# An attention and mixing kernel: GpSimd rotates q and k ahead of splitting v, and the orders of four engines change

## The chip, the cores and the metric

One NeuronCore of one Trainium2 chip runs the whole kernel. The metric is the time of one execution in microseconds (us), measured on the device; less is better. The core has five engines that run their own instruction streams and meet through semaphores: TensorE (PE; its weight loads are shown as PEld), VectorE (DVE), ScalarE (ACT), GpSimd (POOL) and SyncE (SP), which here only issues DMA transfers.

## What is computed

```python
# q, k, v: (4, 8, 576, 64) float32; H * D = 512
q_rot, k_rot = rotate(q), rotate(k)            # rotary positions: halves times cos and sin
scores = (1 / sqrt(D)) * q_rot @ k_rot^T
attn = exp(scores - max(scores))
attn = attn / (sum(attn) + 1e-9)
x = (attn @ v)  as (4, 576, 512)
xk, xr = mu * x + (1 - mu) * x_prev            # mu_k and mu_r; x_prev is x shifted by one row
x = sigmoid(xr @ w_r) * (relu(xk @ w_k)**2 @ w_v)
u = x + token mixing of x (w_tok1, relu, w_tok2)
out = u + relu(u @ w_ch1) @ w_ch2
```

All inputs and the output are float32. Products are made in three matmuls of rounded high parts and low rests, so most operands are split into a "hi" (rounded, by ScalarE or GpSimd) and a "lo" (the rest, by VectorE or GpSimd).

## The kernel before, in words

The 32 heads go through a software pipeline of slots. In slot h, the kernel scores head h, weighs head h - 1 (turns its probabilities and multiplies them with v), and prepares head h + 1 (transposes its rotated q and k and splits them). GpSimd rotates q and k still earlier. Two slots, `slot(it, 0)` and `slot(it, 1)`, make one turn of the loops over `it`; slots 0, 1, 30, 31 and the last one, which only weighs, are written outside of the loop. Behind the 32 heads come the gated part, the token mixing and the channel mixing, which the change doesn't touch.

The order of an engine's work in a slot is written by hand as a string, lines 65 to 67. A letter is a kind of work and a digit is which tile or unit of it:
- For TensorE (`ORDER`): T turns a unit of the last head's probabilities (8 units, line 606), S scores one of five tiles of queries (line 588), P prepares the next head: P0 transposes q and the last keys (lines 572, 573) and P1 the other keys (line 577), V weighs a unit (lines 620 and 626). V0 reads v unsplit (`raw_v`), V1 to V7 the split `v_pair`. All V wait for the split of v, by a wait in front of V0.
- For ScalarE (`ACT_ORDER`): H rounds a turned unit (line 850), P0 to P3 round the transposed keys and q (lines 816, 820, 824), E is the exponential of a tile with its sum (line 837), O copies the low part of an output span (line 855), v rounds v of this slot's head (line 861, into `v_pair`).
- For VectorE (`DVE_ORDER`): I adds 1e-9 to the last head's sums and inverts them (lines 1078, 1080), M is the maximum of a tile (line 1054), L the rest of a turned unit (line 1071), P0 to P3 the rests of q and k (lines 1027, 1033, 1038), O adds an output span into `xT` (line 1088).

Two score tiles and two turned units have PSUM banks at a time, so S2 waits for E0, S3 for E1, T2 for H0, T3 for L1, and so on.

GpSimd's order is the function `slots` (lines 514 to 523). `split_v` (line 490) makes the low part of v and waits for ScalarE's v. `rotate` (lines 481 to 486) makes the rotated q and k of the head two ahead; it waits for the load of that head and for the transposes (P1) of the head that used the same buffer. TensorE's P0 waits for it. `split_w1_hi` and `split_w1_lo` (lines 498, 501) split a piece of the gated part's weights; the first waits until n loads of weights have landed. `scale_x` (line 507) multiplies two finished heads in `xT` by the inverse sums that were read back.

SyncE issues all transfers of the loop in one order, `slots` of its block: for each head `sums_out` (line 376: the inverse sums, 5 x 128 numbers of 4 bytes, into DRAM; waits for the inversion), `next_v` (lines 366 and 368: v of the head two on; waits until the weighing of V0 and the split have freed the buffer), `sums_back` (line 384: reads the sums back, repeated over 64 partitions; waits for their landing in DRAM and, for even heads, for `scale_x` of the pair before), on one side of the pair a load of weights (line 372, the first ten pairs), and `next_qk` (lines 362, 363: q and k of the head four or five on; waits for the rotation that frees the buffer). A wait holds everything behind it in the queue:

```python
def sums_back(it, kk, first=False):
    sp.wait_ge(sums_stored, it * 32 + (16 * kk + 16))
    if i == 0 and not first:
        sp.wait_ge(x_scaled, it)
    sp.dma_start(rb[...], sum_rows[...]).then_inc(rb_in, 16)
```

Of the kernel before, what the change touches and what calls it, by code (L numbers as in the profile page):

```python
# [14 lines left out]
def attention_rwkv_mixer(nc: bass.Bass, q, k, v, mu_k, mu_r, w_k, w_v, w_r,  # L15
# [43 lines left out]
    def steps(text):  # L59
        return [(x[0], int(x[1])) for x in text.split()]  # L60
# [1 line left out]

    ORDER = steps("T0 T1 S0 P0 S1 T2 V0 T3 V1 S2 T4 V2 T5 S3 P1 T6 V3 T7 S4 V5 V4 V6 V7")
    ACT_ORDER = steps("H0 H1 P0 P1 P2 H2 E0 H3 E1 H4 O0 H5 E2 v0 H6 H7 P3 E3 O1 E4")
    DVE_ORDER = steps("I0 M0 L0 L1 M1 P0 L2 P1 L3 M2 P2 L4 O0 L5 M3 L6 L7 M4 P3 O1")

    LAST_ORDER = steps("T0 T1 V0 V1 T2 T3 V2 T4 V3 K0 T5 V4 K1 T6 V5 K2 T7 V6 K3 V7")
    LAST_ACT_ORDER = steps("H0 H1 X0 H2 X1 H3 O0 X2 H4 X3 H5 X4 H6 X5 H7 X6 O1 X7")  # L70
# [6 lines left out]
    with ExitStack() as ctx:  # L77
# [223 lines left out]
        def upto(it, kk, n, c):  # L301

            return it * (2 * n) + (n * kk + c)
# [21 lines left out]
        def rope_half(rot, by_cos, by_sin, j, h):  # L325

            half = D // 2
            a = by_cos[:, j, :, h * half:(h + 1) * half]
            b = by_sin[:, j, :, (1 - h) * half:(2 - h) * half]
            if j == 0:  # L330
                return rot[:, 0:NT, h * half:(h + 1) * half], a, b
            return (rot[:, :, :, h * half:(h + 1) * half], a.unsqueeze(2).to_broadcast([P, NT, 2, half]),
                    b.unsqueeze(2).to_broadcast([P, NT, 2, half]))

        def both(table):
            return table[:, :, :].unsqueeze(1).to_broadcast([P, 2, NT, D])
# [131 lines left out]
        @block.gpsimd  # L468
        def _(pool):
            g = nc.gpsimd  # L470
            pool.wait_ge(zeros_ready, 1)
            g.affine_select(out=ident[:, :], in_=ident[:, :], compare_op=ALU.not_equal, fill=1.0, base=0,
                            pattern=[[-1, P]], channel_multiplier=1).then_inc(ident_ready, 1)

            def rotate(it, i, kk, first):

                pool.wait_ge(qk_in[i], it * 64 + (64 * (kk // 2) + 64))
                if not first:
                    pool.wait_ge(prep_turned, upto(it, kk - 2, 2, 2))
                    pool.wait_ge(k_roped, upto(it, kk, 1, 0))  # L480
                g.tensor_tensor(times_cos[:, :, :, :], raw_qk[i][:, :, :, :], both(cos), ALU.mult).then_inc(rope_step, 1)  # L481
                g.tensor_tensor(times_sin[:, :, :, :], raw_qk[i][:, :, :, :], both(sin), ALU.mult).then_inc(rope_step, 1)  # L482
                pool.wait_ge(rope_step, upto(it, kk - 1, 2, 2))
                for j, (rot, done) in enumerate(((rot_q[i], q_roped), (rot_k[i], k_roped))):
                    g.tensor_tensor(*rope_half(rot, times_cos, times_sin, j, 0), ALU.subtract)
                    g.tensor_tensor(*rope_half(rot, times_cos, times_sin, j, 1), ALU.add).then_inc(done, 1)  # L486

            def split_v(it, i, kk):
                pool.wait_ge(v_hi_ready, upto(it, kk, 1, 1))
                g.tensor_tensor(v_pair[i][:, :, D:P], raw_v[i][:, :, 0:D], v_pair[i][:, :, 0:D], ALU.subtract).then_inc(v_lo_ready, 1)  # L490

            def piece(it):
                return bass.ds(it * PIECE, PIECE)

            def split_w1_hi(it, n):

                pool.wait_ge(w1_in, n * 16)
                g.tensor_copy(w1_hi[:, piece(it)], w1_raw[:, piece(it)]).then_inc(w_hi, 1)

            def split_w1_lo(it):  # L500
                g.tensor_tensor(w1_lo[:, piece(it)], w1_raw[:, piece(it)], w1_hi[:, piece(it)], ALU.subtract).then_inc(w_lo, 1)  # L501

            def scale_x(p):
                pool.wait_ge(span_out, p * 4 + 4)
                pool.wait_ge(rb_in, p * 32 + 32)
                at = bass.ds(p * COLS + 1, S)
                g.tensor_tensor(xT[:, at], xT[:, at], rb[:, :], ALU.mult).then_inc(x_scaled, 1)

            pool.sem_inc(q_roped, 1)
            pool.sem_inc(k_roped, 1)  # L510
            pool.wait_ge(tables_in, 32)
            rotate(0, 1, 1, True)

            def slots(it, n, scaling):
                split_v(it, 0, 0)
                rotate(it, 0, 2, False)
                split_w1_hi(it, n)
                pool.wait_ge(w_hi, it + 1)
                split_v(it, 1, 1)
                split_w1_lo(it)  # L520
                rotate(it, 1, 3, False)
                if scaling:
                    scale_x(it - 1)

            slots(0, 1, False)
            with pool.Fori(1, N_WV) as it:
                slots(it, it + 1, True)
            with pool.Fori(N_WV, HEADS // 2 - 1) as it:
                slots(it, N_WV, True)
            last = HEADS // 2 - 1  # L530
            split_v(last, 0, 0)
            for n in range(last, HALF_UNITS):
                split_w1_hi(n, N_WV)
                pool.wait_ge(w_hi, n + 1)
                split_w1_lo(n)
                if n == last:
                    split_v(last, 1, 1)
                if n == last + 2:
                    scale_x(last - 1)
            scale_x(last)  # L540


            for n, (size, sources, hi, lo, _) in enumerate(TOK_UNITS):
                pool.wait_ge(tok_w_in[n], 16 * len(sources))
                g.tensor_copy(hi, stage_w[:, n, 0:size]).then_inc(w_hi, 1)
                pool.wait_ge(w_hi, HALF_UNITS + n + 1)
                g.tensor_tensor(lo, stage_w[:, n, 0:size], hi, ALU.subtract).then_inc(w_lo, 1)


            with pool.Fori(0, B) as b:  # L550
                for j, (hi, lo) in enumerate(((wc1_hi, wc1_lo), (wc2_hi, wc2_lo))):
                    at = bass.ds(b * STAGE, STAGE)
                    pool.wait_ge(ch_w_hi, b * 2 + (j + 1))
                    g.tensor_tensor(lo[:, at], stage_w[:, j, :], hi[:, at], ALU.subtract).then_inc(w_lo, 1)  # L554
# [3 lines left out]
        def _(pe):  # L558
# [95 lines left out]

            def slot(it, kk, scoring=True, weighing=True, preparing=True, order=ORDER):

                i = kk % 2
                first_score = isinstance(it, int) and it == 0 and kk == 0
                for what, n in order:
                    if what == "S" and scoring:  # L660
                        score(it, i, kk, n, first_score)
                    elif what == "T" and weighing:
                        turn(it, 1 - i, kk - 1, n, weighing == "first")
                    elif what == "V" and weighing:
                        weigh(it, 1 - i, kk - 1, n, weighing == "first")
                    elif what == "K":
                        if n == 0:
                            pe.wait_ge(w_lo, KD * FF // PIECE)
                        gated_k(0, n)
                    elif what == "P" and preparing:  # L670
                        prepare(it, 1 - i, kk + 1, n)
# [139 lines left out]
        def _(act):  # L811
# [69 lines left out]

            def slot(it, kk, scoring=True, weighing=True, preparing=True, first=False, order=ACT_ORDER):
                i = kk % 2
                for what, n in order:
                    if what == "X":
                        if n == 0:
                            wait_for_room(act)
                            act.wait_ge(omu_ready, 1)
                            act.wait_ge(x_scaled, KD)
                        mix2(0, 0, n, after=False)  # L890
                    if what == "E" and scoring:
                        exponent(it, i, kk, n)
                    elif what == "H" and weighing:
                        hi_part(it, kk - 1, n)
                    elif what == "O" and weighing:
                        copy_o_lo(it, 1 - i, kk - 1, n)
                    elif what == "v" and scoring:
                        values_hi(it, i, kk, first)
                    elif what == "P" and preparing:
                        prep(it, 1 - i, kk + 1, n)  # L900
# [120 lines left out]
        def _(dve):  # L1021
# [86 lines left out]

            def slot(it, kk, scoring=True, weighing=True, preparing=True, first=False, order=DVE_ORDER):
                i = kk % 2  # L1110
# [190 lines left out]
```

## Time and profile before

| | us |
|---|---|
| median of 3 runs | 1166.11 (1163.17 to 1166.35) |
| the profiled execution, its own time | 1165.27 |
| its span, first to last instruction | 1163.1 |
| busy: TensorE | 1016.8 |
| busy: VectorE | 636.4 |
| busy: ScalarE | 537.0 |
| busy: GpSimd | 298.0 |

The span is counted from the first to the last instruction of the profiled execution; its time holds 2.17 us more. "Busy" leaves out waits. The granted clock (PEclk) is the share of 2.4 GHz that TensorE was given, so 0.50 is 1.2 GHz. In the timeline a bracket behind a row gives the idle time of the engine before it and what ended it.

### The profile page before, as it was taken

The numbers are of one execution on the slowest core, as the hardware profiler recorded it, in microseconds if no ns is written. First come the engines' busy times: TensorE is split into PE (matmuls) and PEld (weight loads), VectorE is DVE, ScalarE is ACT, GpSimd is POOL, SyncE is SP. The second block draws the span as 40 slices with busy tenths as digits, with TensorE's granted clock in tenths as the row PEclk, the third lists the DMA queues.
The fourth block names the chain that finished last, engine by engine and source line by source line (L and its number), as shares of the span: only waits on it lengthen the run. The fifth ranks groups of instructions, "written<-read, shape, count | busy, mean of one in ns | idle before, by whom it ended". The sixth has DMA issues, their size and how long they took to land.

```text
span 1163.1 us, 21141 instructions
## 1 busy us (share of the span) xinstructions
PE 1016.8 (87%) x6976; PEld 961.7 (83%) x6976; DVE 636.4 (55%) x1232; ACT 537.0 (46%) x1280; POOL 298.0 (26%) x291
## 2 busy tenths in 40 slices
PE   4877777777777777879999999999999999999998
PEld 3766666666776666779999999988899999999997
DVE  5666666667666666779777777744522122212211
ACT  3666666666666666764444434435312112211210
POOL 4454555554544455442000000024200000000000
PEclk9888888998888888889999999999999999999999
DMA  3122222222222121111000000003000000000000
GB/s 81 38 60 58 60 57 52 53 60 60 60 42 42 40 39 31 22 47 62 1 0 0 0 0 0 0 28 108 28 1 21 21 1 20 20 20 0 20 20 20
DMA packets 93629, 37.70 MB, mean 32 GB/s; under 512 B 84000, under 2 KB 84896, under 8 KB 93600
## 3 DMA queue, kind: packets, MB, share of 16 engines
q1 hardware_dynamic: 93312, 37.00, 12.9%
q10 hardware_dynamic: 288, 0.33, 0.1%
q8 instruction: 16, 0.26, 0.1%
q14 instruction: 13, 0.11, 0.1%
HBM read 32.51 MB, written 4.80 MB: 32 GB/s over the span
## 4 chain that ended last, share of the span: by engine, by line
PE 66%; issue 14%; POOL 11%; ACT 5%; DVE 3%; POOLq 0%; DMA 0%; ACTq 0%; SPq 0%; DVEq 0%
PE psum L635 17%; PE psum L637 17%; PE psum L636 17%; PE psum L588 4%; POOL times_cos L481 3%; POOL times_sin L482 3%; PE psum L620 3%; PE psum L606 3%; POOL w_lo L501 2%; PE psum L572 2%; PE psum L626 2%; ACT probs L837 1%; ACT pT_hi L850 1%; POOL rot_q L486 1%; PE psum L723 1%
## 5 line engine op out<-in xcount | busy, mean ns | idle before, releaser
L1054 DVE TENSOR_REDUCE neg_max<-psum 128x1 f32<-128x576 f32 (+1 forms) x160 | 120.5, 753 | 120.8 <-PE psum L588 112.0
L1003 ACT ACTIVATE h_hi<-psum 128x288 fp32r<-128x288 f32 x96 | 39.5, 411 | 245.8 <-PE psum L637 245.8
L606 PE MATMUL psum<-ident,probs 128*128 128x128 f32 x800 | 137.9, 295 | 2.4 <-issue 2.3
L572 PE MATMUL psum<-ident,rot_q 128*128 128x128 f32 x96 | 24.7, 387 | 117.6 <-issue 109.1
L850 ACT ACTIVATE pT_hi<-psum 128x320 fp32r<-128x320 f32 (+3 forms) x224 | 100.7, 450 | 42.7 <-PE psum L606 38.9
L837 ACT ACTIVATE probs<-psum,neg_max 128x576 f32<-128x576 f32 (+1 forms) x160 | 118.0, 737 | 3.6 <-DVE neg_max L1054 2.0
L606 PEld LDWEIGHTS psum<-ident,probs 128*128 128x128 f32 x800 | 103.3, 151 | 17.9 <-issue 8.6
L588 PE MATMUL psum<-kT_hi,qT 128*128 128x288 f32 x320 | 111.3, 360 | 7.4 <-DVE kT_lo L1038 5.6
L572 PEld LDWEIGHTS psum<-ident,rot_q 128*128 128x128 f32 x96 | 14.4, 192 | 123.7 <-issue 123.7
L635 PE MATMUL psum<-u_hi,wc_hi 128*128 128x288 f32 x384 | 114.3, 298 | 0.2 <-DVEq L1239 0.2
L635 PE MATMUL psum<-h_hi,wc_hi 128*128 128x288 f32 x384 | 113.7, 296 | 0.0
L636 PE MATMUL psum<-u_lo,wc_hi 128*128 128x288 f32 x384 | 113.3, 295 | 0.0
L636 PE MATMUL psum<-h_lo,wc_hi 128*128 128x288 f32 x384 | 113.3, 295 | 0.0
L637 PE MATMUL psum<-h_hi,wc_lo 128*128 128x288 f32 x384 | 112.9, 294 | 0.0
L637 PE MATMUL psum<-u_hi,wc_lo 128*128 128x288 f32 x384 | 112.9, 294 | 0.0
L1245 DVE SCALAR_TENSOR_TENSOR h_lo<-psum,h_hi 128x288 fp32r<-128x288 f32 x96 | 43.9, 457 | 125.8 <-ACT h_hi L1003 125.8
L1071 DVE TENSOR_TENSOR pT_lo<-psum,pT_hi 128x320 fp32r<-128x320 f32 (+1 forms) x160 | 84.4, 528 | 29.0 <-ACT pT_hi L850 25.6
L588 PE MATMUL psum<-kT_lo,qT 128*128 128x288 f32 x320 | 99.3, 322 | 0.0
L554 POOL TENSOR_TENSOR wc_lo<-stage_w,wc_hi 128x1536 f32 x8 | 28.4, 3570 | 270.1 <-ACT wc_hi L961 270.1
L626 PE MATMUL psum<-pT_hi,v_pair 128*128 128x320 f32 (+1 forms) x256 | 89.4, 357 | 5.2 <-DVE pT_hi L1071 2.8
L1252 DVE TENSOR_TENSOR outT<-psum,xT 128x288 f32<-128x288 f32 x32 | 14.6, 458 | 124.9 <-PE psum L637 124.9
L588 PEld LDWEIGHTS psum<-kT_hi,qT 128*128 128x128 f32 x320 | 67.7, 212 | 14.1 <-issue 9.1
(127 smaller groups left out, 2943.0 us busy)
## 6 DMA issues: line engine op xcount, KB each, us to landing
stage_w<-in_moe_w_ch_dram SPq DMA_DIRECT2D x8, 768.0 KB, 4.2
rb<-sum_rows SPq DMA_DIRECT2D x32, 144.0 KB, 3.6
out_dram<-stage_out SPq DMA_DIRECT2D x8, 576.0 KB, 3.7
raw_qk<-in_q_dram SPq DMA_DIRECT2D x32, 128.0 KB, 2.5
raw_qk<-in_k_dram SPq DMA_DIRECT2D x32, 128.0 KB, 2.3
raw_v<-in_v_dram SPq DMA_DIRECT2D x32, 128.0 KB
w_raw<-in_moe_w_k_dram SPq DMA_DIRECT2D x4, 512.0 KB, 5.0
w_raw<-in_moe_w_v_dram SPq DMA_DIRECT2D x4, 512.0 KB, 4.9
```

Source lines behind the costliest of these rows:

```text
L572: t.transpose(prep_bank[:, p * P:(p + 1) * P], rot_q[i][:, 2 * p:2 * p + 2, :].rearrange("p a d -> p (a d)"), ident[:, :])
L588: ins = t.matmul(bank[:, x, 0:HALF], qT[i][:, tile * P:(tile + 1) * P], keys[:, x * HALF:(x + 1) * HALF], start=(n == 0), stop=(n == 1))
L606: ins = t.transpose(bank[:, at:at + P], probs[i][:, tile, at_key:at_key + P], ident[:, :])
L626: ins = t.matmul(o_bank[:, 0:width], v_pair[i][:, j, :], x, start=(j == 0 and a == 0), stop=(j == FULL))
L635: t.matmul(dst, a, x, start=start, stop=False)
L636: t.matmul(dst, a, y, start=False, stop=False)
L637: return t.matmul(dst, b, x, start=False, stop=stop)
L837: a.activation(probs[i][0:m, tile, :].rearrange("p (x n) -> p x n", x=2), score_banks[(NT * kk + tile) % 2][0:m, :, 0:HALF], ACT.Exp, bias ...
L850: a.activation(dst, bank, ACT.Copy).then_inc(turn_hi, 1)
L1054: d_.tensor_reduce(neg_max[0:m, at:at + 1], score_banks[at][0:m, :, 0:HALF], AX.XY, ALU.max, negate=True).then_inc(maxed, 1)
L1071: d_.tensor_tensor(dst, bank, src, ALU.subtract).then_inc(turn_lo, 1)
L1245: d_.scalar_tensor_tensor(out=h2_lo[:, f, :], in0=psum[:, f % 4, 0:HALF], scalar=0.0, in1=h2_hi[:, f, :], op0=ALU.max, op1=ALU.subtract).t ...
```

## The change

GpSimd's turn is reordered: rotation (of the even head), the rounded piece of weights, then the split of v; then the rotation of the odd head, the rest of the weights' piece, the scaling of x, and last the other split of v. ScalarE rounds v behind H3 in place of E2's back, and O0 moves ahead of E1. TensorE's V2 moves ahead of T4 and S2, P1 ahead of S3, S3 ahead of V3, T6 and T7 stand side by side, and V4 comes before V5. VectorE's M1, P0, P1, L2 and O0 are reordered to match. In the loop GpSimd waits for `it` loads of weights and no longer for `it + 1`. SyncE's order stays.

```diff
-    ORDER = steps("T0 T1 S0 P0 S1 T2 V0 T3 V1 S2 T4 V2 T5 S3 P1 T6 V3 T7 S4 V5 V4 V6 V7")
-    ACT_ORDER = steps("H0 H1 P0 P1 P2 H2 E0 H3 E1 H4 O0 H5 E2 v0 H6 H7 P3 E3 O1 E4")
-    DVE_ORDER = steps("I0 M0 L0 L1 M1 P0 L2 P1 L3 M2 P2 L4 O0 L5 M3 L6 L7 M4 P3 O1")
+    ORDER = steps("T0 T1 S0 P0 S1 T2 V0 T3 V1 V2 T4 S2 T5 P1 S3 V3 T6 T7 S4 V4 V5 V6 V7")
+    ACT_ORDER = steps("H0 H1 P0 P1 P2 H2 E0 H3 v0 O0 E1 H4 H5 E2 H6 H7 P3 E3 O1 E4")
+    DVE_ORDER = steps("I0 M0 L1 P0 P1 L2 M1 L3 P2 O0 M2 L4 L5 M3 L6 L7 M4 P3 O1")
...
             def slots(it, n, scaling):
-                split_v(it, 0, 0)
                 rotate(it, 0, 2, False)
                 split_w1_hi(it, n)
+                split_v(it, 0, 0)
                 pool.wait_ge(w_hi, it + 1)
-                split_v(it, 1, 1)
+                rotate(it, 1, 3, False)
                 split_w1_lo(it)
-                rotate(it, 1, 3, False)
                 if scaling:
                     scale_x(it - 1)
+                split_v(it, 1, 1)
...
             with pool.Fori(1, N_WV) as it:
-                slots(it, it + 1, True)
+                slots(it, it, True)
```

## Rows read from the trace of the kernel before

**Rows 1.** The page: the span, and the busy time of each engine.
```profile
span 1163.1 us, 21141 instructions
...
PE 1016.8 (87%) x6976; PEld 961.7 (83%) x6976; DVE 636.4 (55%) x1232; ACT 537.0 (46%) x1280; POOL 298.0 (26%) x291
```

**Rows 2.** Stretches: busy us of PE, PEld, DVE, ACT, POOL, PEclk, DMA share, GB/s.
```profile
269.25:299.91 30.66, 22.98 (x144) 20.48 (x144) 20.41 (x41) 20.22 (x51) 16.23 (x17) 0.89 0.24 57
```

**Rows 3.** The waits of the whole span: us in total, times, longest.
```profile
PE psum L572 <- issue: 109.1, 30, 4.3
```

**Rows 4.** The timeline, start and duration in us: GpSimd and TensorE around a pause.
```profile
299.91 0.88 POOL L490 TENSOR_TENSOR v_pair<-raw_v,v_pair 128x320 fp32r<-128x320 f32 x1 [6.79 <-ACT v_pair L861]
...
305.66 0.86 POOL L486 TENSOR_TENSOR rot_k<-times_cos,times_sin 128x320 f32<-128x320 f32 x1
...
306.62 0.87 PE L572 MATMUL psum<-ident,rot_q 128*128 128x128 f32 x3 [2.98 <-issue]
```

**Rows 5.** Stretches behind that pause, columns as in rows 2.
```profile
306.00:310.00 4.00, 3.38 (x13) 3.20 (x14) 1.24 (x3) 1.94 (x5) 0.52 (x1) 0.57 0.05 16
310.00:316.00 6.00, 6.00 (x47) 5.57 (x45) 5.32 (x12) 5.34 (x15) 1.99 (x3) 1.00 0.65 171
```

**Rows 6.** ScalarE's timeline: the copies of a preparation, and the last scoring slot.
```profile
307.74 0.22 ACT L816 ACTIVATE kT_hi<-psum 128x64 fp32r<-128x64 f32 x1 [3.50 <-PE psum L573]
307.99 0.89 ACT L820 ACTIVATE qT<-psum 64x256 fp32r<-64x256 f32 x2
...
315.29 0.60 ACT L824 ACTIVATE kT_hi<-psum 128x512 fp32r<-128x512 f32 x1
...
488.01 0.58 ACT L850 ACTIVATE pT_whole<-psum 128x512 f32<-128x512 f32 x1
...
490.83 0.73 ACT L837 ACTIVATE probs<-psum,neg_max 128x576 f32<-128x576 f32 x1
...
493.75 0.47 ACT L861 ACTIVATE v_pair<-raw_v 128x320 fp32r<-128x320 f32 x1
...
497.29 0.58 ACT L850 ACTIVATE pT_whole<-psum 128x512 f32<-128x512 f32 x1
```

**Rows 7.** SyncE's waits (total, times, longest), and a load's landing, median us.
```profile
SPq L383 <- POOL xT L507: 160.1, 15, 11.6
SPq L384 <- DMA sum_rows<-rsums: 97.4, 14, 8.9
...
raw_qk<-in_q_dram SPq DMA_DIRECT2D x32, 128.0 KB, 2.5
```

**Rows 8.** SyncE's issues: ns min/median/max, first and last start; then its timeline.
```profile
L376 SPq DMA_DIRECT2D sum_rows<-rsums x32: 390/426/587, 30.5 to 500.7; - x32
L384 SPq DMA_DIRECT2D rb<-sum_rows x32: 465/468/478, 39.9 to 509.4; - x32
...
293.25 0.48 SPq L384 DMA_DIRECT2D rb<-sum_rows  x1
...
296.88 0.40 SPq L376 DMA_DIRECT2D sum_rows<-rsums  x1
...
306.58 0.47 SPq L384 DMA_DIRECT2D rb<-sum_rows  x1
...
310.61 0.44 SPq L376 DMA_DIRECT2D sum_rows<-rsums  x1
...
419.63 0.41 SPq L376 DMA_DIRECT2D sum_rows<-rsums  x1
...
431.01 0.47 SPq L384 DMA_DIRECT2D rb<-sum_rows  x1
...
478.00 0.59 SPq L376 DMA_DIRECT2D sum_rows<-rsums  x1
```

**Rows 9.** VectorE's inversion of the sums: ns min/median/max, first and last start.
```profile
L1080 DVE RECIPROCAL rsums<-rsums x32: 187/190/192, 25.7 to 497.7; 128x5 f32<-128x5 f32 x32
```

**Rows 10.** A stretch in which only v and sums are under way, columns as in rows 2.
```profile
300.00:306.00 6.00, 3.34 (x24) 2.75 (x22) 4.93 (x10) 4.14 (x10) 5.92 (x7) 1.00 0.06 12
```

## The prediction

> **What bounds the kernel now.** I read the page first: TensorE, the best-used engine, is busy for 87% of 1163.1 us [rows 1]. Then the stretches. The change touches only the attention part, a loop over pairs of heads. One turn takes 30.66 us, and in it VectorE works 20.4, ScalarE 20.2 and GpSimd 16.2 us [rows 2]. So no engine is full, and what each waits for decides. The list of waits names it: TensorE stands 109.1 us in 30 waits, 3.64 us a head, before it transposes q and k of the next head [rows 3]. The timeline shows what it waits for. GpSimd has stood 6.79 us for ScalarE's rounding of v, which comes late in a slot. It splits v at 299.91, only then rotates, ends the last piece of rot_k at 306.52, and TensorE's transposes start at 306.62, after 2.98 us of idleness [rows 4]. The granted clock is 0.57 from 306 to 310 us, so 1.2 GHz for some 3.4 of the 4 us behind that pause, and 1.00 (2.4 GHz) from 310 to 316, with TensorE at work all through [rows 5]. The loop that sets the time is thus: v rounded (ScalarE), v split, q and k rotated (GpSimd), transposes (TensorE), and on through the slot.
>
> **Part 1, GpSimd's order.** The rotation of a head needs its loads and the transposes of the head two before. Ahead of the split it no longer waits for this slot's v. GpSimd has 16.2 us of work for a pair, so it can run a slot ahead and the transposes find their input there. Removed: 3.64 us a slot and the low clock behind it. The split of v now stands behind the rotation and, for the odd head, behind the scaling of x; the next slot's weighing is the first to need it.
>
> **Part 2, v earlier on ScalarE, and the order of S, V, L and E.** Nothing is added. What would a slot take if only the engines counted? The last scoring slot, which prepares no head and has no pause, shows it: ScalarE from 488.01 to 497.29, 9.28 us, nearly without idleness. The four copies of a preparation add 0.22, 0.89 (two) and 0.60 us, less 0.1 of overlap: 10.9 us [rows 6]. VectorE has 10.2, half of 20.4 [rows 2]. With some 0.4 for the turn of the loop, an estimate, I get 11.3 us a slot.
>
> **Part 3, the wait for weights** comes one load earlier. It lies on GpSimd, off the path once the rotation is ahead, and I give it nothing of its own. The cover is GpSimd's idle third.
>
> **What is late next: SyncE's queue.** Its order isn't changed, and it is serial: send a head's sums (L376), load v of the head two on (L366, L368), wait for the sums' landing, read them back (L384), load q and k, send the next sums. Today it has slack: 160.1 us in 15 waits for the scaling of x, one a pair, and 97.4 us in 14 waits for the landing of the sums [rows 7]. With faster engines the first shrinks and the second comes at every head. Its size: sums sent at 296.88, read back at 306.58, 9.70 us. Of the loop's twelve such landings from 82 us on, the last is 419.63 to 431.01; their mean is 9.63, the longest 11.4. The very last one, at 500.7 and 509.4, has no load ahead of it and still takes 8.7 [rows 8]. From the read back to the next sums there are 4.03 us on one side (306.58 to 310.61, weights among the loads) and 3.63 on the other (293.25 to 296.88) [rows 8]. A pair thus costs the queue 2 x 9.63 + 4.03 + 3.63 = 26.9 us, or 13.5 us a head. That is more than the engines' 11.3 and less than today's 15.2 (30.5 to 500.7 for 31 steps [rows 8]). My forecast is that this queue becomes the bound. For even heads the landing is hidden today behind the wait for x. I take 9.63 for them too, since the only even head that shows it, the first (30.5 to 39.9 [rows 8]), has 9.4. Bounds: 8.7 and 11.4.
>
> **The sum.** Head 0's sums go out at 30.5 today, because the queue stood before the load of head 4, which waits for a rotation; they are inverted by 25.9 [rows 9]. So then 26.0, read back at 35.4 (9.4 as today), head 1's sums at 39.1. Then 13 turns of 26.92 (the last four have no weights to load and are a little shorter; I count them alike), 350.0, and two heads without loads of q and k at 9.63 + 0.47 (a read back's issue [rows 8]), 20.2. Head 29's sums go out at 409.3. Today they go out at 478.00 [rows 8]: gain 68.7.
>
> The end: today ScalarE begins the slot after the last scoring one at 497.29, 19.3 us behind head 29's sums. Then v of head 31 must land first. No wait shows how long that takes behind the sums' own transfer. A load of this size alone lands in 2.5 us from its issue [rows 7], some 4.8 after the sums' issue. But from 300 to 306 us, when only such a v and the sums are under way, the engines still trickle at 12 GB/s [rows 10]; a load of 160 KB isn't over at 300. I take 9.7. Behind the rounding of v ScalarE has 3.5 us of its present tail (493.75 to 497.29) and the five pieces that now come behind v rather than ahead (490.83 to 493.75, 2.9) [rows 6]. 9.7 + 6.5 = 16.2, gain 3.1 (8.0 with v at 4.8 us, 0.8 with v at 12). All behind attention is untouched. The last scaling of x hangs on the queue's last read back, which then comes some 30 us behind head 29's sums (20.2 + 9.6), as today (509.4 less 478.0).
>
> Gain 68.7 + 3.1 = 71.8 us. The profiled execution took 1165.27 us, 0.84 below the median of 1166.11: 1165.3 - 71.8 = 1093 us.
>
> The Trainium skill ("DMA: Bandwidth & Descriptors", "Queues, rings and completion order") has a DMA's semaphore increment land only after every earlier write of that DMA engine. By that v lands no sooner than the sums ahead of it and the sum stays 1093; without it, with v at 4.8 us, it would be 1089. By that rule, the trickle agrees.
>
> **Rivals.**
> 1. *Engines only.* If the landing of the sums doesn't hold the queue, a slot is 11.3 us. 31 slots from about 25 us on end at 375 instead of 497.3, 122 us less: 1043. For it: SyncE's waits are all hidden today. Against it: every landing that can be read is 8.7 us or more, one with nothing ahead. It takes a landing under some 7.5 us (11.3 less 3.8). Chance 0.06. The same page ("Anatomy of one DMA", for GpSimd's path) gives a DMA a fixed cost of about 2.0 us. By that the queue would turn far inside the engines' slot and the time would be 1043; the trace disagrees, with 8.7 at the least.
> 2. *The queue, but slower.* Landings with the weights ahead of them are longer, or the scaling of x, behind a read back and a rotation, comes late for the weighing. Each us on 28 landings is 28 us: 1124 to 1160. Chance 0.10.
> 3. *Slower than before, by the clock.* TensorE works 11.5 us a slot [rows 2], some 1.6 of them extra, from about 3.3 us at the low level, so 9.9 at 2.4 GHz. If short pauses spread over the slot kept it at 1.2 GHz throughout, a slot would take 19.8 us and 30 slots 30 x (19.8 - 15.3) = 135 us more: 1300. It decides from 5.4 us of extra work a slot on, so 10.8 us at the low level. Against it: today the low level follows one pause of 3 us or more and ends while work goes on [rows 4, 5]. Chance 0.03.
> 4. *Nothing.* Another wait as long takes its place, for instance a landing of 11.5 us at every head: within 0.3% of 1166. Chance 0.02.
>
> **Numbers.** The queue as computed has 0.79. Its own range: 28 landings of 8.7 rather than 9.63 (-26), v early (-5), shorter last turns (-3): 1059. The 14 even ones at 11.4 (+25), v late (+2): 1120. I give 1055 to 1124; it leaves out rival 1 and most of 2, 3 and 4. About 0.3% is what a measurement of this kernel can tell from no change. Faster 0.94, same 0.02, slower 0.04.
>
> **What would show it.** TensorE's 109 us before L572 are gone. SyncE waits for the sums' landing at nearly every head, some 200 us in all, and little for the scaling of x. ScalarE's v_pair (L861) waits for raw_v, about 2 us a slot, and TensorE waits before a score (L588) instead. Sums are sent every 13 to 13.5 us, and a pair takes 26 to 27 us. The part behind attention is as long as before. I am wrong if a pair takes about 22.6 us with slack in the queue, if the landing itself changes, or if TensorE's work a slot grows with the clock low.

## The result, and the profile after

The changed kernel takes 1096.45 us (median of 4 runs, 1095.86 to 1097.79) against 1166.23 us before in the same comparison: a ratio of 0.940 with a 95% interval of 0.938 to 0.943. The prediction said 1093 us. The profiled execution of the changed kernel is the run of 1097.79 us, with a span of 1095.7. A later comparison, on another chip or at another time, gave 1077.9 for the same kernel (below); the prediction's reasons have to hold for both.

The page of the changed kernel: the span, the busy times, the granted clock in 40 slices, and the first lines of the chain that ended last.

```profile
span 1095.7 us, 21136 instructions
...
PE 997.6 (91%) x6976; PEld 942.4 (86%) x6976; DVE 634.7 (58%) x1232; ACT 533.6 (49%) x1280; POOL 298.3 (27%) x291
...
PEclk9988988988989999999999999999999999999999
...
PE 57%; DMA 22%; SPq 8%; issue 7%; DVE 3%; ACT 2%; POOL 1%; POOLq 0%; DVEq 0%; ACTq 0%
```

Nothing got less work, but for TensorE's 19 us: fewer of its instructions run at the low clock (mean granted clock 0.967 against 0.943). What went are waits. The chain that ended last is now 22% DMA and 8% SyncE's queue.

The waits of the changed kernel, all engines, then SyncE's own (us in total, times, longest):

```profile
POOL xT L507 <- DMA rb<-sum_rows: 63.9, 12, 6.9
ACT v_pair L861 <- DMA raw_v<-in_v_dram: 57.5, 22, 5.7
...
PE psum L588 <- ACT probs L837: 48.9, 20, 5.2
...
PE psum L572 <- DVE rot_k L1148: 8.9, 1, 8.9
```

```profile
SPq L384 <- DMA sum_rows<-rsums: 175.3, 26, 9.8
SPq L383 <- POOL xT L507: 12.5, 5, 6.5
```

The 30 waits before L572 [rows 3] are gone. One is left, at the start of the kernel, before the loop. SyncE's two waits have changed places: 160.1 us for the scaling of x became 12.5, and 97.4 us for the landing of the sums became 175.3 [rows 7]. ScalarE now waits for v, which it did not before, and TensorE stands before a score because the exponentials behind v are late.

SyncE's timeline, start and duration in us, over two heads of the changed kernel and the start of a third:

```profile
218.55 0.44 SPq L376 DMA_DIRECT2D sum_rows<-rsums  x1
219.24 1.47 SPq L366 DMA_DIRECT2D raw_v<-in_v_dram  x1
220.92 1.19 SPq L368 DMA_DIRECT2D raw_v<-in_v_dram  x2
230.08 0.48 SPq L384 DMA_DIRECT2D rb<-sum_rows  x1
...
233.72 0.40 SPq L376 DMA_DIRECT2D sum_rows<-rsums  x1
...
242.90 0.47 SPq L384 DMA_DIRECT2D rb<-sum_rows  x1
...
246.80 0.44 SPq L376 DMA_DIRECT2D sum_rows<-rsums  x1
```

From sums to sums there are 15.17 and 13.08 us, of which 11.5 and 9.2 go by from the issue of the sums to their landing, when the queue may go on. Over the heads 1 to 27 a pair takes 27.0 us (39.73 to 390.68 in 13 turns). The chain between 200 and 260 us is this queue and nothing else:

```profile
207.59 6.51 issue
214.10 0.47 SPq L384
...
218.55 11.51 DMA sum_rows<-rsums
230.08 0.48 SPq L384
...
233.72 9.16 DMA sum_rows<-rsums
242.90 0.47 SPq L384
...
246.80 12.04 DMA sum_rows<-rsums
```

### The profile page after: what moved, and what is told of

Same layout as the page of the kernel before. It is cut to its first block, busy times and chain, and to the rows that moved or that the text cites. A ratio compares the mean times of both kernels' runs of the same rounds, so it can differ in the third digit from the quotient of the medians.

```text
span 1095.7 us, 21136 instructions
## 1 busy us (share of the span) xinstructions
PE 997.6 (91%) x6976; PEld 942.4 (86%) x6976; DVE 634.7 (58%) x1232; ACT 533.6 (49%) x1280; POOL 298.3 (27%) x291
## 4 chain that ended last, share of the span: by engine, by line
PE 57%; DMA 22%; SPq 8%; issue 7%; DVE 3%; ACT 2%; POOL 1%; POOLq 0%; DVEq 0%; ACTq 0%
DMA sum_rows<-rsums 19%; PE psum L635 18%; PE psum L637 18%; PE psum L636 18%; SPq L363 3%; SPq L362 3%; SPq L384 1%; DMA raw_qk<-in_k_dram 1%; DMA raw_v<-in_v_dram 1%; PE psum L723 1%; PE psum L799 1%; PE psum L588 1%; DVE k_lo L1173 1%; ACT stage_out L998 0%; SPq L368 0%
## 5 line engine op out<-in xcount | busy, mean ns | idle before, releaser
L588 PE MATMUL psum<-kT_hi,qT 128*128 128x288 f32 x320 | 113.9, 369 | 53.6 <-ACT probs L837 48.9
L606 PE MATMUL psum<-ident,probs 128*128 128x128 f32 x800 | 131.5, 292 | 8.1 <-DVE pT_lo L1071 3.8
L606 PEld LDWEIGHTS psum<-ident,probs 128*128 128x128 f32 x800 | 99.0, 149 | 28.2 <-DVE pT_lo L1071 17.6
L850 ACT ACTIVATE pT_hi<-psum 128x320 fp32r<-128x320 f32 (+3 forms) x224 | 96.6, 446 | 30.0 <-PE psum L606 28.1
L626 PE MATMUL psum<-pT_hi,v_pair 128*128 128x320 f32 (+1 forms) x256 | 86.5, 348 | 13.3 <-DVE pT_hi L1071 9.0
L1071 DVE TENSOR_TENSOR pT_lo<-psum,pT_hi 128x320 fp32r<-128x320 f32 (+1 forms) x160 | 81.7, 527 | 17.7 <-ACT pT_hi L850 14.8
L635 PE MATMUL psum<-xk_hi,w_hi 128*128 128x288 f32 x256 | 76.0, 297 | 0.5 <-DVE xk_lo L1107 0.3
L635 PE MATMUL psum<-k_hi,w_hi 128*128 128x288 f32 x256 | 75.8, 296 | 0.0
```

The source lines that it names most:

```text
L588: ins = t.matmul(bank[:, x, 0:HALF], qT[i][:, tile * P:(tile + 1) * P], keys[:, x * HALF:(x + 1) * HALF], start=(n == 0), stop=(n == 1))
L606: ins = t.transpose(bank[:, at:at + P], probs[i][:, tile, at_key:at_key + P], ident[:, :])
L626: ins = t.matmul(o_bank[:, 0:width], v_pair[i][:, j, :], x, start=(j == 0 and a == 0), stop=(j == FULL))
L635: t.matmul(dst, a, x, start=start, stop=False)
L850: a.activation(dst, bank, ACT.Copy).then_inc(turn_hi, 1)
L1071: d_.tensor_tensor(dst, bank, src, ALU.subtract).then_inc(turn_lo, 1)
```

## The experiments

My theory: SyncE's serial queue, held at each head by the wait for the sums' landing in DRAM, sets the time of a head. Rivals: the engines and their waits for each other set it and the queue only follows; the rotation was not what the change freed; or the number of transfers counts wherever they stand. The runs came in three comparisons: the first four together on one chip, the next four on another, the last four again on that other chip, some ten minutes later. The changed kernel itself was timed only in the last one, so the middle four are read against its 1077.9 us there. The first four lie beside 1096.45 with more reserve: their chip has no time for the changed kernel, but the landings in the third of them are like those of the result's profile (means of 9.8 and 10.0 us for odd and even heads, against 9.6 and 10.1).

### The read back behind q and k

```diff
                 if not start:
                     sums_out(it, -1)
                     next_v(it, 0)
-                    sums_back(it, -1)
                 if w is not None:
                     load_w1(w, it, first, tiles)
                 if more:
                     next_qk(it, 0)
+                if not start:
+                    sums_back(it, -1)
                 sums_out(it, 0)
                 next_v(it, 1)
-                sums_back(it, 0, first=start)
                 if more:
                     next_qk(it, 1)
+                sums_back(it, 0, first=start)
```

> The changed kernel, with SyncE reading the sums back behind the load of q and k instead of ahead of it, so that the wait for their landing holds one transfer less. Theory (the serial queue of SyncE is the bound, 13.2 us a head): a head costs the queue only the landing, 9.6 to 10.5 us, the read back and the next issue, 1.1 us, together 10.7 to 11.6, about what the engines need (11.3); 29 heads by some 1.9 us less: 1035 to 1055 us. Rival (engines or their waits for each other set the 13.2 us a head, and SyncE only follows): no change, 1090 to 1100.

Measured 1060.1 us (1054.0 to 1063.3), ratio 0.910 (0.908 to 0.913). That is 36 us less than the result's 1096.45, from moving two transfers in SyncE's queue alone. The engines' orders are those of the changed kernel, so the rival falls. It ends 5 us above the range that I gave. A pair took 24.0 us, not 21.4 to 23.2. Two things show why. From the sums to their read back 10.5 us (odd heads) and 11.0 us (even heads) now go by, where I had given 9.6 to 10.5, and SyncE still waits 98.1 us in 24 waits for landings. And in places the read back itself takes 10.3 us, and GpSimd's scaling of x, the split of v behind it and the weighing wait for it. First the chain, then SyncE's timeline:

```profile
189.85 10.27 DMA rb<-sum_rows
201.48 0.87 POOL v_pair L491
202.57 2.07 PE psum L621 x4
```

```profile
189.85 0.47 SPq L384 DMA_DIRECT2D rb<-sum_rows  x1
190.54 0.42 SPq L376 DMA_DIRECT2D sum_rows<-rsums  x1
```

### The same edit in the kernel before

> The kernel before with the same one edit in SyncE's order. Theory (before, the rotation behind the split of v is the bound and SyncE's queue has slack): no change, 1158 to 1168 us, TensorE's waits before L572 stay near 109 us. Rival (the queue was the bound of the kernel before too): faster by 20 us or more.

Measured 1164.1 us, ratio 0.9989 (0.9979 to 1.0). The edit that gives 36 us in the changed kernel gives 1 us in the kernel before. The queue had slack, as the prediction read it from its waits. SyncE's time simply moved to another wait, for the rotation:

```profile
SPq L362 <- POOL rot_k L487: 261.9, 29, 10.8
SPq L383 <- POOL xT L508: 22.8, 2, 11.6
SPq L384 <- DMA sum_rows<-rsums: 19.3, 3, 8.2
```

### GpSimd's order alone

```diff
-    ORDER = steps("T0 T1 S0 P0 S1 T2 V0 T3 V1 V2 T4 S2 T5 P1 S3 V3 T6 T7 S4 V4 V5 V6 V7")
+    ORDER = steps("T0 T1 S0 P0 S1 T2 V0 T3 V1 S2 T4 V2 T5 S3 P1 T6 V3 T7 S4 V5 V4 V6 V7")
```

and likewise the old orders of ScalarE and VectorE, with the changed `slots` of GpSimd.

> The changed GpSimd order alone, with the three old orders of TensorE, ScalarE and VectorE (v rounded late). Theory: the rotation is a slot ahead all the same, and the queue sets 13.2 us a head; v is wanted later in the slot, so the engines can follow the queue a little closer: 1088 to 1102 us, TensorE's waits before L572 gone. Rival (the earlier rounding of v is what frees the rotation, the order of GpSimd by itself is not enough): 1120 or more.

Measured 1098.9 us (1094.4 to 1100.5), ratio 0.942 (0.939 to 0.944): the interval overlaps that of the whole change, though the two were timed in different comparisons. TensorE's waits before L572 are gone but for one of 8.6 us. SyncE waits 196.7 us in 28 waits for landings, and a pair takes 27.4 us. So GpSimd's order, with its changed count of loads, is enough for about this change's whole gain: the queue sets the pace here too. What the three other orders bring once the queue is fast wasn't tried.

### The three orders alone

The reverse: the kernel before with the changed `ORDER`, `ACT_ORDER` and `DVE_ORDER`, GpSimd's order as before.

> The three changed orders (v rounded early) with the old order of GpSimd. Theory: the split of v and the rotation behind it start about 6 us earlier in a slot and end about when the next slot wants them; the wait for the weights in between still delays the odd head's rotation by a us or so: 1096 to 1120 us, TensorE's waits before L572 below 40 us. Rival (only GpSimd's order matters): near 1160.

Measured 1113.8 us (1111.5 to 1114.7), ratio 0.955 (0.953 to 0.957). Rounding v earlier shortens the same loop from the other end and brings some three quarters of the gain by itself (51.7 us, where GpSimd's order brings 66.6 in the same comparison). The pauses that are left are longer than I expected, 56 us rather than below 40, and GpSimd's waits for the weights (78.6 us) lie in front of the odd head's rotation:

```profile
PE psum L572 <- issue: 55.9, 15, 7.1
POOL w_hi L498 <- DMA w_raw<-in_moe_w_v_dram: 37.2, 4, 10.1
POOL w_hi L498 <- DMA w_raw<-in_moe_w_k_dram: 24.1, 3, 8.6
POOL w_hi L498 <- DMA w_raw<-in_moe_w_r_dram: 17.3, 2, 8.6
```

### The old count in the wait for the weights

```diff
-                slots(it, it, True)
+                slots(it, it + 1, True)
```

> The changed kernel with the old count in the wait for the weights (it + 1 loads instead of it). Theory (the wait is off the path, as the prediction has it): GpSimd waits for a load issued 10 us behind the odd head's sums and landing 5 to 6 us later, ahead of the split of v that the next weighing wants; the weighing shifts against the queue but the queue's turn stays 26.9 us: 1096 to 1110 us. Rival (the split of v behind that wait becomes the bound): 10 pairs by 4 us or more, 1130 and up.

Measured 1103.5 us (1102.6 to 1104.2), ratio 0.947 (0.945 to 0.949). Beside 1077.9 for the changed kernel on this chip that is 25.6 us more. The number falls into the theory's range only because that range started from 1096; read as what the count costs, both sides missed: neither "off the path" nor 40 us. GpSimd stands up to 18 us for a load that it doesn't need yet, and the split of v is behind it; the next weighing waits for the split nine times, once in each pair that loads weights:

```profile
PE psum L620 <- POOL v_pair L490: 55.5, 9, 8.6
POOL w_hi L498 <- DMA w_raw<-in_moe_w_v_dram: 51.8, 4, 13.4
POOL w_hi L498 <- DMA w_raw<-in_moe_w_k_dram: 45.4, 3, 18.3
```

So the small edit of the count is needed by the new order of GpSimd: beside it, the old count costs 25.6 us.

### The sums in runs of 20 bytes

```diff
-    sum_rows[bass.ds(it * 2 + kk, 1), :].rearrange("o (t p) -> p (o t)", p=P)
+    sum_rows[bass.ds(it * 2 + kk, 1), :].rearrange("o (p t) -> p (o t)", p=P)
-    sum_rows[bass.ds(it * 2 + kk, 1), 0:S].to_broadcast([D, S])
+    w_ch1[bass.ds(it * 2 + kk, 1), 0:S].to_broadcast([D, S])
```

> The changed kernel, with the sums written to DRAM in 128 runs of 20 bytes instead of 640 of 4 bytes, and the read back taken from a row of w_ch1 of the same size: the scaling by the sums is left out in effect (x is multiplied by other numbers). Order, waits and count of transfers stay. Theory (the sums' slow landing holds SyncE's queue): if the landing falls to 3 to 5 us the queue turns in some 8 us a head and the engines bind at 11.3: 1040 to 1050 us, ScalarE no longer waits for raw_v. Rival (the landing is a fixed latency of a write to DRAM, whatever its pieces): landing still 9 us, 1090 to 1100.

Measured 1020.6 us (1019.5 to 1020.9), ratio 0.876 (0.875 to 0.878), 57 us below the changed kernel on this chip. SyncE's timeline:

```profile
205.79 0.38 SPq L376 DMA_DIRECT2D sum_rows<-rsums  x1
...
209.53 0.47 SPq L384 DMA_DIRECT2D rb<-in_moe_w_ch_dram  x1
...
216.59 0.38 SPq L376 DMA_DIRECT2D sum_rows<-rsums  x1
```

SyncE's sums, and the profile's own figure for their landing:

```profile
L376 SPq DMA_DIRECT2D sum_rows<-rsums x32: 361/376/383, 24.0 to 353.8; - x32
...
DMA to landing us min/median/max: 1.5/1.5/3.0
```

The same 2.5 KB now land in 1.5 us (median; 3.0 at most). The read back still goes out 3.7 us behind the sums, but only because the issues of v stand between: SyncE waits once for a landing (2.1 us, at the last head). From these sums to the next there are 10.8 us, and what SyncE waits for is VectorE, 108.0 us in 32 waits for the inverted sums. What is left is the engines' own pace. A stretch of one pair (columns as in rows 2):

```profile
200.00:221.40 21.40, 20.17 (x145) 17.88 (x143) 20.05 (x41) 19.97 (x51) 16.43 (x17) 1.00 0.31 81
```

TensorE and VectorE are busy for 94% of it and ScalarE for 93%, and TensorE's granted clock is 1.00 in it. A pair takes 21.4 us, 10.7 a slot, where I had estimated 11.3. The time is 20 us under the lower end of my range. This edit frees more than the queue's wait: with fewer pieces the other transfers land sooner too (the read back, here of another tensor in DRAM, in 3.1 us, median, instead of 4.2 in the changed kernel on this chip), so the 57 us are not the price of the held queue alone. The runs that move transfers and leave the pieces as they are, above and below, tell that part.

The Trainium skill ("DMA: Bandwidth & Descriptors", "Rules for kernel authors") says that a strided last dimension becomes one descriptor per element. The packets of the queue agree with it. The first line is from the page of the changed kernel, the second from that of this run (packets, MB, share of 16 engines):

```profile
q1 hardware_dynamic: 93312, 37.00, 14.8%
...
q1 hardware_dynamic: 76928, 37.00, 13.8%
```

That is 16384 packets fewer, 512 for each of 32 heads, which is 640 less 128. From the issue of 640 pieces of 4 bytes to the read back that waits for them 7.9 to 12.2 us go by in the runs that keep SyncE's order.

### Two extra small loads, on the path and under the wait

```diff
...
+            def extra(k):
+                for n in range(2):
+                    sp.dma_start(spare[:, 2 * k + n, :], w_tok1[0:P, n * 8:(n + 1) * 8]).then_inc(spare_in, 16)
```

Once behind `sums_back` of every head, once between `next_v` and `sums_back`.

> The changed kernel with two more small loads (4 KB each, never used) for each head, issued by SyncE right behind the read back, so on the queue's path. Theory (serial queue): each costs its issue, 0.5 to 0.6 us, 29 heads: plus 28 to 36 us, 1124 to 1134. Rival (the queue isn't the bound): plus less than 5 us.

> The same two loads for each head, but issued between the load of v and the wait for the sums' landing, so in the time that the queue waits anyway. Theory: their issue is hidden under the landing; plus 0 to 8 us (they may delay the landing itself a little): 1096 to 1104. Rival (more transfers cost by their number, through the DMA engines, wherever they stand): the same plus 28 to 36 us as behind the read back.

Measured 1108.2 us (1102.9 to 1109.1) behind the read back, and 1087.0 us (1084.6 to 1088.6) under the wait. Beside the 1096.45 that both expectations started from, the first looks like a third of its price and the second like a gain. Extra work can hardly be a gain, so the next comparison asked what the changed kernel takes on this chip.

> The changed kernel itself, timed again beside the next three on the same chip, since the two extra loads under the landing had made it faster (1087 against 1096.5 us in another comparison): 1094 to 1099 us. If it comes out near 1087, that difference was between comparisons and not between kernels.

> The changed kernel with only the 128 bytes of spare memory per partition put in front, no extra loads: all later tiles are moved by 128 bytes. If the place of the tiles is what made the extra loads' kernel faster, 1085 to 1090 us; if the extra transfers behind v did it, 1094 to 1099.

> The kernel with two extra small loads under the landing again: 1084 to 1090 us if its gain is real.

| kernel, on the same chip | us (median) | ratio, 95% interval | a pair in the queue, us |
|---|---|---|---|
| changed kernel | 1077.9 | 0.926 (0.925 to 0.927) | 25.8 |
| with the 128 bytes of spare memory only | 1078.9 | 0.927 (0.925 to 0.929) | 25.9 |
| two loads under the wait, again | 1086.7 | 0.932 (0.931 to 0.934) | 26.4 |
| two loads behind the read back (the comparison before) | 1108.2 | 0.950 (0.947 to 0.952) | 28.0 |

So the difference was between comparisons and not between kernels: the changed kernel is 18.6 us faster there, while the kernel before takes the same 1164 to 1166 us in all of them. Against the right base the loads on the path cost 30.3 us, inside the 28 to 36 expected, and those under the wait 8.8 to 9.1, a little over the 0 to 8. The queue's turns say the same: 14 turns of 28.02 - 25.83 = 2.19 us are 30.7 us. The loads under the wait lengthen the landing of odd heads by 0.6 us, from 8.9 to 9.5 and 9.6 (means of 14 heads).

The changed kernel's SyncE waits on this chip, beside 175.3 and 12.5 us in the result's profile:

```profile
SPq L384 <- DMA sum_rows<-rsums: 162.5, 26, 8.4
SPq L383 <- POOL xT L507: 9.6, 4, 6.0
```

The landings have means of 8.94 and 9.50 us (odd and even heads) against 9.57 and 10.10 in the result's profile. 0.6 us on 28 landings is 17 of the 18.6 us. The kernel before hides the even landings and is bound elsewhere, so its time doesn't show this.

### A version that holds nothing

```diff
...
+                    next_v(it, 0)
+                    if w is not None:
+                        load_w1(w, it, first, tiles)
+                    sums_out(it, -1)
+                    sums_back(it, -2, first=isinstance(it, int) and it == 1)
+                    if more:
+                        next_qk(it, 0)
...
+                split_v(it, 1, 1)
                 if scaling:
                     scale_x(it - 1)
-                split_v(it, 1, 1)
```

The other half of the pair likewise, `sums_stored` as one semaphore for even and one for odd heads, and the first and last turns of SyncE written out to match.

> A version meant to beat both: the changed kernel, where SyncE loads v first, then sends the sums of a head, and reads back the sums of the head before (which have landed by then), then loads q and k; a semaphore for the sums of even and odd heads each; GpSimd scales x behind the second split of v. Theory (the held queue is what costs): nothing in the queue waits for a landing any more, the engines bind as in the run with the sums in runs: 1018 to 1035 us. Rival (the transfers' slow landings delay v or q and k all the same, since these are behind or beside the sums): 1045 to 1065, as with the read back behind q and k.

Measured 1044.2 us (1037.6 to 1047.2), ratio 0.895 (0.893 to 0.898). It is the fastest version that computes everything, 34 us under the changed kernel on the same chip, and lies between the theory's range and the rival's. SyncE waits only 10.0 us in 3 waits for a landing of the sums. But the chain has found the next thing, first in the chain of waits, then in GpSimd's timeline:

```profile
213.98 11.07 DMA rb<-sum_rows
```

```profile
199.79 1.21 POOL L514 TENSOR_TENSOR xT<-xT,rb 128x576 f32 x1 [7.60 <-DMA rb<-sum_rows]
...
225.24 1.42 POOL L514 TENSOR_TENSOR xT<-xT,rb 128x576 f32 x1 [9.21 <-DMA rb<-sum_rows]
```

The read back lands in 3.6 us (median) in the kernel before and in 4.4 in the changed one. Here it needs 11.07 when it is issued 0.6 us behind the next head's sums (213.37), whose data it does not read. The rule of the Trainium skill that the prediction weighed ("Queues, rings and completion order") would have it so: a completion comes only after every earlier write of the DMA engine. This row agrees with it. The 10.27 us of the first experiment's read back are another matter: that one went out at 189.85, after the sums ahead of it had landed and 0.69 us ahead of the next ones (190.54), so no write of sums stood before it. Why it took as long isn't shown. GpSimd's rotation stands behind the scaling and SyncE's load of q and k behind the rotation (52.5 us in 17 waits). SyncE also waits 79.5 us in 22 waits until the weighing has freed the buffer of v, which is now the first load of a head. A pair takes 23.5 us instead of 21.4. Sending the sums behind the read back, or in longer runs, would be next; neither was tried.

## Why the prediction was right

**The bound before.** Right. The 109.1 us before L572 are gone with the change and with GpSimd's order alone, and shrink to 55.9 with the early v alone.

**What comes next.** Right, and this carried the number. The queue's turn was put at 26.9 us a pair and is 27.0. That it is so close is partly luck: landings of odd heads have a mean of 9.57 (9.63 taken), but those of even heads, hidden before, have 10.10, and other turns are shorter than counted. The nine turns with weights take 27.6 us each. The four without take 25.5; the prediction called them a little shorter and counted them alike. The sums of head 0 went out at 25.58 (26.0 said), of head 1 at 39.73 (39.1), of head 29 at 411.67 (409.3).

**The end.** Its size was off. ScalarE's timeline of the changed kernel:

```profile
424.79 0.47 ACT L861 ACTIVATE v_pair<-raw_v 128x320 fp32r<-128x320 f32 x1 [1.99 <-DMA raw_v<-in_v_dram]
...
432.63 0.58 ACT L850 ACTIVATE pT_whole<-psum 128x512 f32<-128x512 f32 x1
```

v of the last head was there 13.1 us behind the sums of head 29, which had landed by 422.00, 10.3 us behind their issue. I took 9.7 and gave 12 as the upper end, and the rest of the slot took 7.8 us, not 6.5. Instead of gaining 3.1 us this piece lost 1.7. Behind it the kernel takes 1095.7 - 432.6 = 663.1 us against 665.8 before; that 2.7 us was not in the sum. The granted clock is 1.00 in the first 20 us of it and was 0.83 in the kernel before; whether that makes the 2.7 wasn't tried. Together: 68.7 became 66.3, 3.1 became -1.7, and 2.7 came in. That makes 67.3 of the 67.4 us of the two spans' difference, where 71.8 were said.

**The rivals.** "Engines only" was refused for the right reason, the landing, and what it would give was put too small: the run with the short landing takes 1020.6 us rather than 1043. The engines' floor of 11.3 us a slot was an estimate with 0.4 us for the loop's turn, and that run shows 10.7. "The queue, but slower" is true in small: even heads' sums go out behind a load of weights in the first ten pairs, and their landings have a mean of 10.5 us there (heads 2 to 18) and 9.1 after (heads 20 to 26). The low clock didn't spread: the mean granted clock rises from 0.943 to 0.967. It still follows TensorE's longer pauses. Behind one of 4.41 us the granted clock is 0.50, so 1.2 GHz, from 219.40 to 222.00. The timeline, then the stretch (columns as in rows 2):

```profile
219.40 0.61 PE L588 MATMUL psum<-kT_hi,qT 128*128 128x288 f32 x1 [4.41 <-ACT probs L837]
219.81 0.44 PE L588 MATMUL psum<-kT_lo,qT 128*128 128x288 f32 x1
220.05 0.44 PE L588 MATMUL psum<-kT_hi,qT 128*128 128x288 f32 x1
```

```profile
219.40:222.00 2.60, 2.60 (x11) 2.56 (x12) 1.95 (x4) 1.38 (x5) 1.95 (x2) 0.50 1.05 250
```

**What the agreement is worth.** That 1096.45 lies 3.4 us from 1093 is partly luck. The turn's terms cancel, as shown, and in a later comparison the same kernel takes 1077.9, 15 below the number and well inside the range of 1055 to 1124. The range was made of the landing's bounds, and the landing is what differs.

**Part 3** was given nothing, as "off the path", and that reason is wrong: with the old count the changed kernel takes 25.6 us more, so beside the new order of GpSimd the edit is worth that much. GpSimd's idle third was no cover for a wait of up to 18.3 us in front of a split of v. The total came out all the same, because the sum never counted such a wait.

## What to carry to other kernels

Before an engine's pause is priced, ask what is second: here a transfer queue whose waits were all hidden had a serial turn of 13.5 us a head, and it took some two fifths of what there was to gain (57 of 145 us on the chip where the changed kernel and the one with the short landing were both timed). Sum a queue's own turn from its issues and landings, also where the trace shows it idle. A queue that waits for its own write in the middle of its order holds every load behind it; moving the read back behind the loads was worth some 36 us, and only once the first bound was gone. And write small numbers in long runs: 128 pieces instead of 640 brought the landing from 9 us to 1.5, though only in a kernel that leaves out the scaling by the sums; a complete one wasn't tried.

## What the runs showed of the hardware that was not expected

A transfer of 2.5 KB in 640 pieces of 4 bytes from SBUF to DRAM holds the queue that waits for it for 7.9 to 12.2 us from its issue, and up to 14.0 in the first experiment, where q and k are loaded in between. In 128 pieces of 20 bytes it lands in 1.5 us, 3.0 at most.

The mean of the first differs between comparisons, 8.9 against 9.6 us for odd heads of the same kernel, and moves that kernel from 1096 to 1078 us, while the kernel that hides it stays at 1164 to 1166. Two comparisons on one chip agree (1087.0 and 1086.7 us for the same kernel), which speaks for the chip rather than the hour, but the chip of the result isn't on record.

A read that is issued right behind such a write lands about as late as such a write does: 7.9 to 11.7 us in the four places where it stands in the last version's chain, against a median of 3.6 in the kernel before, though it reads other data. In the first experiment one issued 0.69 us ahead of such a write took 10.27 us too.
